# Expert steps of 256 rows with the weights as stationary operand, in a two-layer mixture-of-experts kernel

## The chip, the cores and the metric

The kernel runs on one core of a Trainium2 chip. The metric is the device time of one execution in microseconds (us); lower is better. Times come from executions on the chip. The profile and its trace are of one such execution, and "clock" is the share of full speed that TensorE's throttle granted.
## What is computed

A decayed linear attention, then an expert layer in which each row goes to its best expert, then one in which each row goes to its two best. Cut to what matters:

```python
x = attention(r, k, v, w, u)                     # 3072 rows of 384
e_idx = argmax(x @ w_gate + modality_bias[modality_id])
for e in range(8):                               # layer 0: one expert for each row
    mask = e_idx == e
    h = maximum(x[mask] @ w1[e], 0)              # w1[e] 384 x 1024
    x1[mask] = gate_w[mask, None] * (h @ w2[e])  # w2[e] 1024 x 384
top2 = two best of (x1 @ w_gate2 + softplus(x1 @ w_noise) * noise)
for e in range(8):                               # layer 1: two experts for each row
    for k in range(2):
        mask = top2[:, k] == e
        out[mask] += top2_w[mask, k, None] * (maximum(x1[mask] @ w1b[e], 0) @ w2b[e])
```

Evaluated for the inputs that are timed, the routing sends 2663 and 409 rows to two experts in layer 0 (none to the other six), and 788, 753, 773, 790, 741, 753, 785 and 761 rows to the eight experts of layer 1. Of the first 1536 rows of layer 0, 1336 go to the first expert.

## The kernel before

**Stages.** The attention runs in 24 chunks of 128 tokens. During its last chunks the kernel finds the expert of the first row and lists that expert's rows among the first 1536, so that five tiles of layer 0 (the early tiles, ET = 5) can be gathered before the routing of all rows is known. Then follow layer 0, the gate of layer 1, its routing tables, and layer 1.

**A tile of an expert layer** is 128 rows of one expert, places without a row being filled up. GpSimd gathers the rows with an indirect DMA (`gather_rows`, L551) into one of two buffers `sx`. TensorE transposes them (`slot_turn`, L1556, three 128x128 blocks). VectorE splits the transposed rows into a rounded part `x_hi` and a remainder `x_lo` (`split_x`, L1344, L1346), with two small operations ahead of it in layer 1 for the row's weight (L1339, L1342). A product is three matmuls: hi by hi, hi by lo, lo by hi (`products`, L1644 to L1646), so the weights too are kept as two parts; `split_piece` makes them in four quarters, on ScalarE (L748), VectorE (L1080) and GpSimd (L618), while the first tile of the run before is computed. A run is all tiles of one expert.

**First product** (`up`, L1648): the rows are the stationary operand and 512 columns of w1 stream past, so a half of the hidden values lies in one bank with rows on partitions. There are 2 halves, 3 blocks of 128 inputs and 3 matmuls, 18 matmuls of 512 columns. ScalarE copies the half out (`hidden_copy`, L802), TensorE transposes it in four blocks (`hidden_turn`, L1665), ScalarE applies the ReLU and rounds (`hidden_high`, L807), and VectorE makes the remainder (`hidden_low`, L1351).

**Second product** (`down`, L1668): the hidden values are stationary, and 384 columns of w2 stream past; 8 blocks and 3 matmuls, 24 matmuls of 384 columns. VectorE copies the result out (`result_copy`, L1359 or L1362) and GpSimd scatters it (L654, L657; in layer 1 each scatter adds to the output and waits for the one before).

**Order on TensorE.** `slot_step` (L1697) does for tile s: the first half of `up` for tile s + 1, the first half of `down` for s, `hidden_turn`, the second half of `up`, `slot_turn` for tile s + 2, the second half of `down`, `hidden_turn`. Ahead of it the sequencer reads two entries of the table `slot_run` (`lookup`, L358), whose values set the weights' addresses in both products; the address registers of `weights[:, bass.ds(at, width)]` are computed between the matmuls (PEldq rows of L1644 and L1645). Every engine runs the same steps in `pairs` (L317): some of them written out, then a loop over four steps (L324), then a loop (L1721) in which each step stands under a condition (L1723) since the number of tiles is known only at run time.

**VectorE in the first tiles.** Between the splits of the first tiles VectorE does the routing of layer 0 in small chained operations: `first_counts`, `first_places`, `first_tiles`, `first_slots`, `first_hot` (three parts), `run_order`, `run_experts`, `first_rows`, `slot_tables`, spread over tiles 0 to 2 (`first_step`, L1389).

Of the kernel before, what the change touches and what calls it, by code (L numbers as in the profile page):

```python
# [16 lines left out]
F32 = mybir.dt.float32  # L17
# [7 lines left out]
P = 128  # L25

def attention_moe_moe(nc, HP, D, w_T, kv_T, small_T, modality_T, modality_bias, w1_1, w2_1, w1_2, w2_2, out):
# [15 lines left out]
    ET, EC, EB = 5, 12, 2  # L44
    NS = [N // P + E - 1 + ET, 2 * N // P + E - 1]
    SURE = [K * N // P for K in TOPK]
    NSX = [n + 4 for n in NS]
    NIN = 3
# [5 lines left out]
    assert ET <= EC <= (B - EB) * NC and ET + 3 <= SURE[0] and EB * NC == 12  # L54
# [4 lines left out]
    with ctx:  # L59
# [8 lines left out]

        y_dram = nc.dram_tensor("moe_rows", [N + NSX[0] * P, CX], F32, kind="Internal").ap()

# [9 lines left out]
        iota_s_row_b, iota_row_b = sb("iota_s_row_b", [P, NSX[1]], BF16), sb("iota_row_b", [P, P], BF16)  # L80
        spare_row = [sb(f"spare_row{l}", [P, NSX[l]]) for l in range(2)]
# [14 lines left out]
        with ExitStack() as early:  # L96
            y_tok = [early.enter_context(nc.sbuf_tensor(f"y_tok{i}", [P, C], F32)) for i in range(2)]
            block_ones = early.enter_context(nc.sbuf_tensor("block_ones", [P, P], F32))

        gx_hi = [sb(f"gx_hi{i}", [P, CC, P], F32R) for i in range(NGT)]  # L100
        gx_lo = [sb(f"gx_lo{i}", [P, CC, P], F32R) for i in range(NGT)]
        gate_split = sb("gate_split", [P, CC, 4 * E], F32R)
# [16 lines left out]
        which = sb("which", [P, NSX[1], 2])  # L119
        row_mix = sb("row_mix", [P, NSX[1]])  # L120
        row_mix2 = sb("row_mix2", [P, 2])
# [11 lines left out]
        with nc.sbuf_tensor("logits_T", [4 * E, GB * P], F32) as logits_T:  # L133
            pass
        low_hot = sb("low_hot", [P, 2 * G, P], BF16)
        high_is = sb("high_is", [P, 2 * G, NSX[1]], BF16)
        high_hot = sb("high_hot", [P, 2 * G, 2, NSX[1]], BF16)
        slot_cmp = sb("slot_cmp", [P, NSX[1], E])
# [27 lines left out]
        code = sb("code", [P, NSX[1]])  # L166
        empty = sb("empty", [P, NSX[1]])
        second = sb("second", [P, NSX[1]])
        idx_tmp = sb("idx_tmp", [P, NSX[1]])
        src_row = [sb(f"src_row{l}", [P, NSX[l]], I32) for l in range(2)]  # L170
        dst_row = [sb(f"dst_row{l}", [P, NSX[l]], I32) for l in range(2)]
# [11 lines left out]
        src_now = [sb(f"src_now{i}", [P, 1], I32) for i in range(2)]  # L183
        dst_now = [sb(f"dst_now{i}", [P, 1], I32) for i in range(2)]
# [36 lines left out]
        sx = [sb(f"sx{i}", [P, CX]) for i in range(2)]  # L221
# [1562 lines left out]
```

## Time and profile before

| | |
|---|---|
| median of 3 executions | 1068.34 us (1067.96 to 1069.35) |
| the profiled execution: time, span of its trace | 1067.66 us, 1065.9 us |
| mean granted clock | 0.952 |
| TensorE busy, its loads busy | 960.4 us (90%), 853.7 us (80%) |
| VectorE, ScalarE, GpSimd busy | 529.6 us, 309.3 us, 354.1 us |
| share of the chain that ended last | PE 84%, DVE 8%, issue 3% |
| stages (us from the start) | attention to 178, layer 0 to 443, gate and routing to 528, layer 1 to 1053, end 1065.9 |

The page gives for each group of instructions its line, engine, operation, tiles, count, then busy time, mean duration of one in ns, and the engine's idle time before them with what ended it. Matmuls are pipelined: the duration of one overlaps the next, so what a matmul costs in a row of them is read from the chain that ended last, which gives each only the time by which it moved the chain on. "Issue" is idle time in which an engine waited for nothing that the profile shows; on TensorE it can be its sequencer.

### The profile page before, as it was taken

What the parts mean: (1) busy time and instruction counts of PE and PEld (TensorE: products, weight loads), DVE (VectorE), ACT (ScalarE), POOL (GpSimd) and SP (SyncE); (2) the same over time, 40 slices, a digit from 0 to 9 for tenths busy, and PEclk for the clock granted to TensorE, in tenths of its full rate; (3) what the DMA queues carried; (4) which work ended last, traced back from release to release, by engine and by line L of the source; (5) the groups of instructions that cost most, each with busy time, mean ns of one, the idle gap of its engine ahead of it and who ended that gap; (6) DMA issues with size and microseconds to landing.
All of it is one profiled execution on the core that took longest, in us unless ns stands there. A gap on an engine that the chain in (4) does not pass through costs nothing.

```text
span 1065.9 us, 25001 instructions
## 1 busy us (share of the span) xinstructions
PE 960.4 (90%) x6314; PEld 853.7 (80%) x6315; DVE 529.6 (50%) x915; ACT 309.3 (29%) x537; POOL 354.1 (33%) x420
## 2 busy tenths in 40 slices
PE   6999998999999999382399999999999999999994
PEld 5888887888888898381278988888888988989884
DVE  8889997755323332147753353533535344363231
ACT  2233242223222222042242242423324242332220
POOL 6333334124222222101633343424424333343322
PEclk9999998899999999776599999999999999999998
DMA  6676861082111111153045252342522525222222
GB/s 234 217 217 221 289 233 45 24 306 78 42 45 37 37 44 41 35 171 119 23 150 155 33 160 44 91 101 44 150 42 36 163 38 162 37 37 44 41 35 37
DMA packets 52997, 108.15 MB, mean 101 GB/s; under 512 B 8336, under 2 KB 34704, under 8 KB 52944
## 3 DMA queue, kind: packets, MB, share of 16 engines
q1 hardware_dynamic: 34656, 71.07, 19.6%
q0 software_dynamic: 14400, 31.55, 14.7%
q10 hardware_dynamic: 3888, 4.89, 1.3%
q8 instruction: 25, 0.41, 0.2%
q14 instruction: 28, 0.23, 0.1%
HBM read 82.67 MB, written 24.82 MB: 101 GB/s over the span
## 4 chain that ended last, share of the span: by engine, by line
PE 84%; DVE 8%; issue 3%; DMA 1%; POOL 1%; ACT 1%; ACTq 0%; POOLq 0%; DVEq 0%; SPq 0%
PE ps L1644 21%; PE ps L1646 20%; PE ps L1645 20%; PE ps L1665 6%; PE ps L1556 3%; PE ps L1518 2%; PE ps L1522 2%; PE ps L1487 2%; PE ps L1464 2%; PE ps L1548 2%; DVE row_mix L1339 1%; PE ps L1570 1%; PE ps L1512 1%; PE ps L1581 1%; DVE grow L882 1%
## 5 line engine op out<-in xcount | busy, mean ns | idle before, releaser
L1351 DVE SCALAR_TENSOR_TENSOR hid_lo<-ps,hid_hi 128x512 fp32r<-128x512 f32 x154 | 106.4, 691 | 292.6 <-ACT hid_hi L807 292.5
L1644 PE MATMUL ps<-weights,hid_hi 128*128 (+1 forms) x616 | 215.6, 350 | 8.2 <-issue 6.7
L1644 PE MATMUL ps<-weights,x_hi 128*128 (+1 forms) x462 | 198.2, 429 | 16.1 <-DVE x_lo L1346 8.6
L1646 PE MATMUL ps<-weights,hid_lo 128*128 (+1 forms) x616 | 208.4, 338 | 0.0
L1645 PE MATMUL ps<-weights,hid_hi 128*128 (+1 forms) x616 | 208.3, 338 | 0.0
L1646 PE MATMUL ps<-weights,x_lo 128*128 (+1 forms) x462 | 184.4, 399 | 0.0
L1645 PE MATMUL ps<-weights,x_hi 128*128 (+1 forms) x462 | 184.2, 399 | 0.0
L802 ACT ACTIVATE h_tok<-ps 128x512 f32<-128x512 f32 x154 | 92.3, 599 | 294.8 <-PE ps L1646 284.1
L807 ACT ACTIVATE hid_hi<-ps 128x512 fp32r<-128x512 f32 x154 | 92.1, 598 | 257.7 <-PE ps L1665 257.7
L657 POOL DMA_INDIRECT out_dram<-sy,dst_now x52 | 92.5, 1778 | 210.6 <-DVE sy L1362 199.8
L1644 PEld LDWEIGHTS ps<-weights,hid_hi 128*128 128x128 f32 x616 | 116.7, 190 | 13.5 <-issue 10.3
L1645 PEld LDWEIGHTS ps<-weights,hid_hi 128*128 128x128 f32 x616 | 116.8, 190 | 3.2
L1644 PEld LDWEIGHTS ps<-weights,x_hi 128*128 128x128 f32 x462 | 87.8, 190 | 37.1 <-issue 22.6
L1646 PEld LDWEIGHTS ps<-weights,hid_lo 128*128 128x128 f32 x616 | 116.4, 189 | 0.0
L1646 PEld LDWEIGHTS ps<-weights,x_lo 128*128 128x128 f32 x462 | 88.0, 191 | 20.6
L1645 PEld LDWEIGHTS ps<-weights,x_hi 128*128 128x128 f32 x462 | 88.1, 191 | 14.2
L1665 PE MATMUL ps<-ident,h_tok 128*128 128x128 f32 x616 | 92.8, 273 | 3.4 <-ACT h_tok L802 3.4
L1665 PEld LDWEIGHTS ps<-ident,h_tok 128*128 128x128 f32 x616 | 76.6, 141 | 10.6 <-ACT h_tok L802 3.9
L654 POOL DMA_INDIRECT moe_rows<-sy,dst_now x25 | 26.4, 1057 | 146.4 <-DVE sy L1359 146.4
L551 POOL DMA_INDIRECT sx<-moe_rows,src_now x55 | 56.5, 1027 | 44.0 <-POOL src_now L548 42.3
L748 ACT ACTIVATE weights<-stage 128x1536 f32 (+1 forms) x40 | 59.0, 1481 | 0.0
L1344 DVE CAST x_hi<-ps 128x384 fp32r<-128x384 f32 x79 | 43.7, 553 | 25.0 <-PE ps L1556 25.0
(281 smaller groups left out, 1151.9 us busy)
## 6 DMA issues: line engine op xcount, KB each, us to landing
stage<-in_moe_w_dram SPq DMA_DIRECT2D x18, 1536.0 KB, 9.4
kv_in<-in_kv_T_dram SPq DMA_DIRECT2D x24, 512.0 KB, 5.7
kv_in<-in_kv_T_dram SPq DMA_DIRECT2D x24, 448.0 KB, 3.5
w_in<-in_w_T_dram SPq DMA_DIRECT2D x24, 258.5 KB, 4.4
out_dram<-zeros SPq DMA_DIRECT2D x25, 192.0 KB, 6.6
x_rows<-y_tok ACTq DMA_DIRECT2D x24, 192.0 KB, 5.2
stage<-moe_rows SPq DMA_DIRECT2D x6, 768.0 KB, 4.6
stage<-in_moe_w_dram SPq DMA_DIRECT2D x2, 768.0 KB, 7.0
```

What stands on the lines that cost most here:

```text
L551: pool.indirect_dma_start(out=sx[u][:, 0:width], out_offset=None, in_=rows, in_offset=bass.IndirectOffsetOnAxis(ap=src_now[u][:, :].bitcas ...
L657: pool.indirect_dma_start(out=out, out_offset=where, in_=sy[u][:, 0:C], in_offset=None, compute_op=ALU.add).then_inc(s_scatter[l][u], 16)
L748: act.activation(weights[:, bass.ds((n % 2) * 4 * WSZ + hi + at, HALF)], raw[:, at:at + HALF], ACT.Copy)\
L802: act.activation(h_tok[:, half * FC // 2:(half + 1) * FC // 2, :], h_ps[half], ACT.Copy)\
L807: act.activation(hid_hi[:, half * FC // 2:(half + 1) * FC // 2, :], hT_ps[half], ACT.Relu)\
L1344: dve.tensor_copy(x_hi[:, :, :], sxT_ps).then_inc(s_xhi[l], 1)
L1351: dve.scalar_tensor_tensor(hid_lo[:, part, :], hT_ps[half], 0.0, hid_hi[:, part, :], ALU.max, ALU.subtract).then_inc(s_hlo[l], 1)
L1556: last = pe.transpose(sxT_ps[:, c, :], sx[u][:, c * P:(c + 1) * P], ident[:, :])
L1644: pe.matmul(out_ps, hi, w_hi, start=first, stop=False)
L1645: pe.matmul(out_ps, hi, w_lo, start=False, stop=False)
L1646: return pe.matmul(out_ps, lo, w_hi, start=False, stop=final)
L1665: last = pe.transpose(hT_ps[half][:, m, :], h_tok[:, half * FC // 2 + m, :], ident[:, :])
```

## The change

A step is now 256 rows (TS = 2 tiles of 128), and the early tiles are three steps (ES = 3, six tiles of 128).

- **First product.** The blocks of w1 are the stationary operand (128 inputs by 128 hidden columns) and the transposed rows of both tiles stream past, 256 columns. The result has hidden columns on partitions, as the second product needs it: `hidden_copy`, `hidden_turn` and the tile `h_tok` go. `up` comes in four quarters `q`, each 2 blocks, 3 inputs' blocks and 3 matmuls; a step has 72 matmuls of 256 columns. Its addresses are constants, so the whole body stands twice in the program, for runs with an even and an odd number, each under a condition on `run_next % 2`.
- **Second product.** As before for each tile of 128, into two banks; the second tile's share stands under a condition on a new table `full`, which is 0 when that tile has no row. `up` is done for 256 rows in any case.
- **Order on TensorE.** Per step: `up` quarter 0 of step s + 1, first half of `down` for the second and then the first tile of s, quarters 1 and 2, `slot_turn` of the first tile of s + 2, quarter 3, second half of `down` for the second tile, `slot_turn` of the second tile of s + 2, second half of `down` for the first tile. The body reads three table entries: `slot_run[s]`, `full[s]`, `slot_run[s + 1]`.
- **Buffers.** `x_hi` and `x_lo` hold 256 rows in one copy: `split_x` waits until all four quarters of the step before are done (`s_h`). The transposed rows use one bank, so the second tile's `slot_turn` waits for the first tile's `split_x` (`s_sxc`). ScalarE's `hidden_high` waits for the half of `down` that reads the same part of `hid_hi` (`s_o`).
- **GpSimd.** Two gathers and two scatters per step; in layer 1 the second scatter waits for the first to land.
- **Routing.** Places, slots and tables are counted in steps of 256; the code tables have two columns for each step. VectorE's order in the first steps changes: `first_hot`, `run_order` and `run_experts` all come ahead of `split_x` of step 2.

The core of the diff:

```diff
+                def up(s, q, run, odd=0):
+                    base = odd * 4 * WSZ + W1_HI
+                    pe.wait_ge(s_lov[l], 2 if isinstance(s, int) and s == 0 else run * 3 + 3)
+                    pe.wait_ge(s_sxc[l], s * TS + TS)
+                    if not isinstance(s, int) or s > 0:
+                        pe.wait_ge(s_hlo[l], (s - 1) * 4 + q + 1)
+                    for a in range(2):
+                        for c in range(CC):
+                            at = base + c * F + (2 * q + a) * P
+                            last = products(h_ps[q][:, a, :], weights[:, at:at + P], weights[:, at + WSZ:at + WSZ + P],
+                                            x_hi[:, c, :], x_lo[:, c, :], c == 0, c == CC - 1)
                     last.then_inc(s_h[l], 1)
-                def hidden_turn(s, half, before=None):
+                def down_second(s, half, run, two):
+                    down_ready(s, half, run)
+                    if two is None:
+                        down(s, half, run, 1)
+                    else:
+                        with pe.If(two > 0):
+                            down(s, half, run, 1)
...
+                    run, two, run_next = run_of(s), second_of(s), run_of(s + 1)
+                    def whole(odd):
...
+                            up(s + 1, 0, run_next, odd)
+                            down_second(s, 0, run, two)
+                            down(s, 0, run, 0)
+                        up(s + 1, 1, run_next, odd)
+                        up(s + 1, 2, run_next, odd)
+                        slot_turn(l, s + 2, j + 1, u, 0)
+                        up(s + 1, 3, run_next, odd)
+                        down_second(s, 1, run, two)
+                        slot_turn(l, s + 2, j + 1, u, 1)
+                        down(s, 1, run, 0)
+                    if early(s + 1):
+                        whole(0)
+                    else:
+                        with pe.If(run_next % 2 < 1):
+                            whole(0)
+                        with pe.If(run_next % 2 > 0):
+                            whole(1)
...
+                def split_x(s, u, t):
+                    part = slice(t * P, (t + 1) * P)
+                    dve.wait_ge(s_sxT[l], s * TS + t + 1)
+                    if not isinstance(s, int) or s > 0:
+                        dve.wait_ge(s_h[l], s * 4)
...
                 def first_step(s, u):
+                    if s == 0:
                         first_hot(0)
+                        first_hot(1)
+                        hidden_low(1, 0)
+                        first_hot(2)
+                        hidden_low(1, 1)
                         run_order()
                         run_experts()
...
+                    split_x(s + 2, u, 0)
+                    split_x(s + 2, u, 1)
+                    result_copy(s, s // 2, u)
```

## Rows read from the trace of the kernel before

**Rows 1.** Windows of the two layers: us, busy and count by engine, clock, DMA.

```profile
189.00:443.00 254.00, 243.26 (x1326) 217.84 (x1325) 99.20 (x195) 64.71 (x103) 65.11 (x100) 0.97 0.21 71
546.00:1053.00 507.00, 494.97 (x2700) 442.71 (x2698) 211.96 (x378) 157.69 (x230) 184.53 (x211) 1.00 0.34 77
```

**Rows 2.** The page's groups of instructions: products, transposes, scatters of both layers.

```profile
L1644 PE MATMUL ps<-weights,hid_hi 128*128 (+1 forms) x616 | 215.6, 350 | 8.2 <-issue 6.7
L1644 PE MATMUL ps<-weights,x_hi 128*128 (+1 forms) x462 | 198.2, 429 | 16.1 <-DVE x_lo L1346 8.6
L657 POOL DMA_INDIRECT out_dram<-sy,dst_now x52 | 92.5, 1778 | 210.6 <-DVE sy L1362 199.8
L1665 PE MATMUL ps<-ident,h_tok 128*128 128x128 f32 x616 | 92.8, 273 | 3.4 <-ACT h_tok L802 3.4
L654 POOL DMA_INDIRECT moe_rows<-sy,dst_now x25 | 26.4, 1057 | 146.4 <-DVE sy L1359 146.4
```

**Rows 3.** The chain that ended last, inside layer 1: start, us, what.

```profile
594.99 0.23 PE ps L1645
...
596.16 0.33 PE ps L1556 x3
...
596.67 0.18 PE ps L1645
...
598.61 0.44 PE ps L1665 x4
```

**Rows 4.** Timeline of the stationary loads behind a transpose: start, duration, instruction.

```profile
703.69 0.19 PEld L1644 LDWEIGHTS ps<-weights,x_hi 128*128 128x128 f32 x1
703.80 0.19 PEld L1645 LDWEIGHTS ps<-weights,x_hi 128*128 128x128 f32 x1
```

**Rows 5.** Timelines of VectorE around one split of the rows in layer 1.

```profile
596.65 0.16 DVE L1339 TENSOR_TENSOR row_mix<-sx,which 128x2 f32<-128x2 f32 x1 [1.24 <-PE ps L1556]
...
597.62 0.56 DVE L1346 TENSOR_TENSOR x_lo<-ps,x_hi 128x384 fp32r<-128x384 f32 x1
```

**Rows 6.** Timelines of ScalarE and TensorE, and between them the sequencer's lookups (L358).

```profile
596.20 0.60 ACT L802 ACTIVATE h_tok<-ps 128x512 f32<-128x512 f32 x1 [1.51 <-PE ps L1646]
...
L358 PEldq TENSOR_LOAD <-slot_run x2: 299/300/300, 597.0 to 597.7; - x2
...
598.87 0.49 PE L1644 MATMUL ps<-weights,x_hi 128*128 x1
```

**Rows 7.** By line, the sequencer's address computations (590.1 to 591.1) and branches (428 to 436).

```profile
L1645 PEldq FUSED_REGOPS  x4: 46/46/46, 590.2 to 591.0; - x4
...
L1723 PEldq COMPARE_BRANCH  x12: 208/208/210, 428.9 to 434.9; - x12
```

**Rows 8.** What TensorE waited for in layer 0 (first row) and layer 1.

```profile
PE ps L1644 <- issue: 9.0, 7, 6.7
...
PE ps L1644 <- DVE x_lo L1346: 7.0, 6, 1.2
PE ps L1644 <- issue: 3.5, 11, 0.8
PE ps L1644 <- DVE hid_lo L1351: 1.5, 1, 1.5
```

**Rows 9.** Windows around two waits of TensorE; the clock is the third number from the end.

```profile
236.00:240.00 4.00, 2.39 (x14) 1.85 (x13) 0.00 (x0) 2.38 (x4) 1.21 (x3) 1.00 1.07 394
...
188.50:195.00 6.50, 6.00 (x17) 4.76 (x18) 5.64 (x21) 0.63 (x2) 1.36 (x3) 0.50 0.12 30
```

**Rows 10.** A window of layer 0's first tiles: busy time by engine.

```profile
190.50:216.50 26.00, 25.75 (x147) 23.03 (x148) 19.57 (x53) 6.84 (x11) 4.58 (x7) 0.91 0.10 32
```

**Rows 11.** The instruction fetches of one engine on the page: packets, MB, share.

```profile
q8 instruction: 25, 0.41, 0.2%
```

**Rows 12.** GpSimd in the routing of layer 1; issues of its scatters, median us to landing.

```profile
510.27 5.60 POOL L611 TENSOR_TENSOR high_hot<-high_is,tile_no 128x1416 bf16<-128x1416 bf16 x1 [1.57 <-DVE high_is L1299]
...
out_dram<-sy,dst_now POOLq DMA_INDIRECT x52, 4.4
```

More of the change, by code:

```diff
@@ L165, in attention_moe_moe @@
         split_later = [sb(f"split_later{l}", [P, NSX[l]], I32) for l in range(2)]
[L166 to L171, printed above, removed]
+        full = [sb(f"full{l}", [P, NSX[l]], I32) for l in range(2)]
+        code = sb("code", [P, NTX[1]])
+        empty = sb("empty", [P, NTX[1]])
+        src_row = [sb(f"src_row{l}", [P, NTX[l]], I32) for l in range(2)]
+        dst_row = [sb(f"dst_row{l}", [P, NTX[l]], I32) for l in range(2)]
         index_b, first_idx = sb("index_b", [P, 1], BF16), sb("first_idx", [P, 1])
@@ L1382, in _ @@
                     loop_ends(1)
-                    hidden_low(0, 0)
-                    split_x(1, 1)
-                    hidden_low(0, 1)
+                    for q in range(3):
+                        hidden_low(0, q)
+                    split_x(1, 1, 0)
+                    hidden_low(0, 3)
+                    split_x(1, 1, 1)
                     dve.wait_ge(s_table[1], 3)
@@ L1648, in up @@
-                def up(s, half, run, before=None):
-                    base = (run % 2) * 4 * WSZ + W1_HI + half * (F // 2)
-                    pe.wait_ge(s_lov[l], 2 if before is None else run * 3 + 3)
-                    pe.wait_ge(s_sxc[l], s + 1)
-                    if before is not None:
-                        pe.wait_ge(s_hc[l], before * 2 + half + 1)
-                    for c in range(CC):
-                        last = products(ps[:, 3 + half, :], x_hi[:, c, :], x_lo[:, c, :],
-                                        base + c * F, F // 2, c == 0, c == CC - 1)
-                    last.then_inc(s_h[l], 1)
@@ L1660, in hidden_turn @@
-                def hidden_turn(s, half, before=None):
-                    pe.wait_ge(s_hc[l], s * 2 + half + 1)
-                    if before is not None:
-                        pe.wait_ge(s_hlo[l], before * 2 + half + 1)
-                    for m in range(FC // 2):
-                        last = pe.transpose(hT_ps[half][:, m, :], h_tok[:, half * FC // 2 + m, :], ident[:, :])
-                    last.then_inc(s_hT[l], 1)
-                def down(s, half, run):
-                    base = (run % 2) * 4 * WSZ + W2_HI
+                    return 0 if early(s) else lookup(pe, slot_run[l], s, E - 1)
@@ new lines, in down @@
+                def down(s, half, run, t):
+                    base = (run % 2) * 4 * WSZ + W2_HI
+                    for m in range(half * FC // 2, (half + 1) * FC // 2):
+                        part = slice(t * P, (t + 1) * P)
+                        last = products(o_ps[t], hid_hi[:, m, part], hid_lo[:, m, part],
+                                        weights[:, bass.ds(base + m * C, C)], weights[:, bass.ds(base + WSZ + m * C, C)],
+                                        m == 0, m == FC - 1)
+                    if t == 0:
+                        last.then_inc(s_o[l], 1)
```

425 lines of the change are left out of this document (218 added, 207 removed).

## The prediction

> **What bounds the kernel now.** I read the windows first: in both layers TensorE is busy for 96% and 98% of the stretch, and no other engine for half [rows 1]. The groups then say how much work that is [rows 2]: 616 and 462 matmuls of each kind are 77 tiles (24 x 3 and 18 x 3 for each, 616 transposes make 8), and the scatters split them in 25 and 52. Mean durations are of no use, since matmuls overlap; the chain gives what each costs in a row of them [rows 3]: 0.233 us for 512 columns, 0.175 for 384, 0.33 for the three transposes of new rows, 0.44 for four of hidden values. A tile is 18 x 0.233 + 24 x 0.175 + 2 x 0.44 + 0.33 = 9.6 us, and 77 of them are 740 of the 761 us of the two windows. So the layers are bound by what TensorE is given, and little is lost between tiles: in layer 1 it waits 12 us [rows 8].
>
> **Part 1, TensorE's work.** All is set against the profiled execution, 1067.7 us (span 1065.9 and 1.8 around it), which is 0.7 under the median. The transposes of hidden values go: 77 x 0.88 = **-67.8 us**. The first product keeps its columns for 256 rows (72 x 256 as 36 x 512). No row shows 256 columns. From 512 to 384 the cost falls in proportion (0.455 and 0.456 ns a column), so 256 give 0.1165 us if loading stays hidden. The bound on the other side is the load: two loads behind a transpose start 0.11 us apart [rows 4], so it fits with 0.006 us to spare. I take 0.1165; if load and stream share anything, 0.125 to 0.13 (over 41 x 72 = 2952 matmuls +25 to +40 us), and nothing makes it cheaper than its columns. A step is then 8.4 us of first product. How many steps: the row counts give 11 and 2 in layer 0, and 4, 3, 4, 4, 3, 3, 4, 3 in layer 1, so 13 and 28. That is 82 tiles' worth of first product for 77: 5 x 4.2 = **+21 us**, since 788, 773, 790, 785 and 2663 rows leave a last step with its second tile empty. The second product stays at 77 tiles. Row transposes: 79 turns become 86, **+2.3**.
>
> **Part 2, the wait between steps.** TensorE's sequencer takes its instructions in order, and a semaphore that isn't there stops it. The rows show it: ScalarE's copy ends at 596.80, the lookups, which stand behind the `hidden_turn` that waits for this copy, begin at 597.0, and the next `up` starts at 598.87 [rows 6]: 2.07 us, two lookups of 0.75 in it. Now that time is just covered by the work queued ahead. In the new order the last wait of a step is `slot_turn` of the second tile. It needs the first tile's `split_x`, which now starts only when quarter 3 is done. Between the end of the transposes (596.16 + 0.33) and the end of `x_lo` (597.62 + 0.56) lie 1.69 us [rows 3, 5]; that is the delay from quarter 3 to this wait in layer 1, and without the two small operations about 1.3 in layer 0. From there the sequencer still has to do: the 2.07 of before; a third lookup, 0.75; the addresses of 12 matmuls, 8 computations at half of the 0.27 us between two of L1645, 1.1 [rows 7]; one branch taken and one not, 0.6 (twelve taken ones and six loop ends fill 428.9 to 434.9 and a bit, 0.38 each; the other I take at 0.22). Sum 4.5 us. What TensorE has meanwhile: second half of `down` twice, 4.2, and 0.33, less the 0.17 by which a next matmul starts before the chain's end (598.87 against 598.61 + 0.44). So it stands still for 1.7 + 4.5 - 4.35 = **1.9 us** at each full step of layer 1, and 1.5 in layer 0. Behind the stopped sequencer everything of TensorE is queued, and ScalarE and VectorE wait for it in turn. Below, this could be nothing, if address computations and lookups went on past an open wait; above, 2.5 if the branches over the long bodies cost more.
>
> Layer 1 has 22 such places (28 steps less the last and the 4 partial ones, and one at the start that has its own order), layer 0 has 8, since its first steps have constant addresses and no lookup: 22 x 1.9 + 8 x 1.5 = **+54 us**. A step without second tile is worse: `slot_turn` comes straight behind quarter 3 and TensorE waits the whole 1.9 us for the split, and then has only 0.33 + 2.1 against 4.5 us, another 2.1. Four times 4.0 and once 3.4: **+19.5**. Loop ends and the conditions of the last loop: **+3.5**.
>
> The Trainium skill, Perfetto Trace Analysis (Tensor Engine Instruction), says that the sequencer can fetch the next instruction once one is pushed into the wait queue, ahead of its semaphores. By that rule the lookups would run under the open wait, this part would be near 0, and the kernel would come to the time of the first rival. The trace speaks against it: the lookups begin only behind the copy's end.
>
> **Part 3, waits that go.** Today's waits at run changes and loop ends go or are in the new figures [rows 8]: 7.0 + 3.5 + 1.5 in layer 1, and in layer 0 9.0 less the 6.7 of its end, and 1.6 for `h_tok` [rows 2]: **-16**. The quarters of the new weights are split in steps twice as long and are off the path; if GpSimd's share slows VectorE they cost 1 us each time, eight times, which I leave to the range.
>
> **Part 4, starts and ends.** Layer 0: VectorE does 19.6 us of work in 26 us [rows 10], most of it routing, and nearly all of it now stands ahead of `split_x` of step 2, which `slot_turn` waits for with half of step 0's `down` behind it. TensorE has about 11 us in that stretch: a stall of 6 us, with the clock at half after it; against that the waits of now and 6.5 us at half clock [rows 9] are there today too. I take +5. A second gather and split ahead of the first `up`: +1 and +1.5. Routing of layer 1: code tables of 70 columns for 59, GpSimd's product 5.6 x 70/59, twice in a row in part [rows 12]: +2.6. The second scatter at the end waits for the first to land, 4.4 [rows 12]; between the layers +1.1. The last step's lookups behind empty loop turns: +3.7 and +0.8. Layer 1's first steps wait less for VectorE: -3. Sum **+17**.
>
> **Sum.** -67.8 + 21 + 2.3 + 54 + 19.5 + 3.5 - 16 + 17 = +33.5, or 1101 us; I say **1102**.
>
> **The rivals.** *Hidden boundaries* (the other side: faster). If the sequencer computes past an open wait, or the chain of 4.5 us is in truth under 2.8, the 54, some 8 of the 19.5 and the 3.5 go: 1102 - 65 = 1037, and with half of it 1070. It decides at 4.5 - 1.9 = 2.6 us: a boundary below that costs nothing. For it speaks that today's 2.07 us are fully covered; against it that five things stand in the chain, each from a row. The change is a gain if the stall is under 0.8 us a step.
>
> *The load binds.* Each stationary block now serves 256 columns instead of 512. With 0.125 to 0.13 us a matmul 1127 to 1142. For it: only 0.006 us of slack; against it: at 384 columns no trace of the load is left.
>
> *The clock falls.* A wait of 1.6 us (4.00 less 2.39 busy) left it at 1.00, while behind several waits close together it was 0.50 for 6.5 us [rows 9]. Stalls of 1.9 us, and two of 2 us around 2.4 us of work in the partial steps, lie between the two. If it fell at every third of 38 boundaries for 3.4 to 6.8 us, each 1.5 to 3 us lost, that is +20 to +40: 1122 to 1142. The Trainium skill, TensorE: Matmul & The Clock Gate (The HAM clock gate), has the clock go down only behind an idle stretch; by that it would stay at full speed; rows 9 agree for one wait and leave open what several do.
>
> *Code that must be fetched.* Each step's body now stands twice and each step jumps over one of them. Today 25 fetches bring 0.41 MB, and no jump shows one [rows 11, 7]. If 15 jumps in 38 met code that isn't there, at 1 to 2 us, +15 to +30: 1117 to 1132. The Trainium skill, Advanced Engine Details and Errata (ISA Cache), gives TensorE 128 KB in blocks of 256 instructions; by my count of some 700 instructions a step a loop of four steps would not fit, so it speaks for this case.
>
> **How the numbers follow.** Stalls as computed 0.42 (1085 to 1118); stalls and one of the three costs on top 0.28 (1112 to 1150); boundaries half hidden 0.12 (1066 to 1085 for a quarter of it, 1050 to 1066 for the rest); boundaries hidden 0.16 (1030 to 1050); the rest 0.02. The range that leaves 2 in 10 out is 1045 to 1145. A measurement of this kernel can tell 0.2%, 2 us, from no change. Faster 0.23, within it 0.02, slower 0.75.
>
> **What would show it.** In the profile after: no group for `h_tok`; first-product matmuls 0.117 us apart on the chain (0.125 or more: the load); 82 x 36 of them; TensorE in layer 1 waiting about 1.9 us at each boundary, put down to issue, with the first matmul of `up` quarter 0 behind it; at partial steps a wait for `x_lo` too; clock near 1.00 in both layers; fetches near twice 25, not many times; a longer end by 4 us. I am wrong if the waits put down to issue in layer 1 are under 20 us in sum (then the sequencer runs past waits), if matmuls of 256 columns cost clearly more than their columns, or if VectorE or ScalarE ends the waits in full steps.

## The result and the profile after

The changed kernel takes 1208.6 us (median of 4 runs, 1203.3 to 1211.6) against 1068.2 for the one before, measured beside it: 1.132 times as long, 95% interval 1.127 to 1.137. I had forecast 1102, with a range of 1045 to 1145. The profiled execution took 1211.6 us, with a span of 1209.6.

First the two layers by windows (columns: stretch, its length, busy time and count of TensorE, its weight loads, VectorE, ScalarE and GpSimd, then granted clock, DMA share, GB/s). The stretches go from the first wait of layer 0 to its last product, and from layer 1's first product to its last boundary:

```profile
207.38:463.92 256.54, 218.50 (x1450) 214.05 (x1450) 85.49 (x169) 32.05 (x51) 60.29 (x77) 0.92 0.22 72
552.84:1186.04 633.20, 508.86 (x3384) 496.90 (x3385) 225.82 (x429) 102.51 (x140) 186.92 (x170) 0.91 0.31 70
```

The same stretch of layer 1 took 520.3 us before (from 528.55 to 1048.80). So of the 143.7 us that the span grew by, 113 lie in layer 1, 21 up to the end of layer 0, 3 in the routing between them and 6.5 at the end. TensorE's busy time in layer 1 looks unchanged (505.7 and 508.9), but it is now 80% of the stretch and not 97%, and the clock stands at 0.91 where it was 0.99 ([rows 1] are this reading of before, in a slightly shorter stretch). At half clock a matmul counts twice: half of the busy time at 0.50 is 3.8 us of it before and 36.6 after. Without that TensorE has 29.6 us less to do, close to what Part 1 gives for layer 1 (52 x 0.88 us of transposes gone, four half steps of 4.2 us more: 29.0).

What TensorE waited for (us in total, times, longest; the first rows), beside [rows 8]:

```profile
PE ps L1676 <- issue: 126.6, 33, 10.2
PE ps L1588 <- DVE x_lo L1364: 21.7, 12, 5.5
```

"Issue" was 9.0 and 3.5 us before. The profile shows no engine that TensorE waited for there; that it is TensorE's own sequencer is read from the sequencer's rows further down. On the page of the profile, the fetches of instructions and the first product's matmuls (x984 for each of three, 82 tiles' worth, as counted):

```profile
q8 instruction: 108, 1.77, 0.6%
...
L1676 PE MATMUL ps<-x_hi,weights 128*128 128x256 f32 x984 | 300.2, 305 | 129.8 <-issue 119.2
```

108 fetches for 25 [rows 11]. Between one back edge of the loop in layer 1 and the next there are 11 to 13 of them, in each of the four passes after the first; in the kernel before there are none. The chain of work shows one boundary between steps (start, us, what); it is a mild one:

```profile
936.77 0.18 PE ps L1678
936.95 1.59 issue
938.53 0.38 PE ps L1676
938.91 0.12 PE ps L1677
```

TensorE stands for 1.59 us. VectorE's timeline and the sequencer's rows show what it stood for:

```profile
933.54 0.56 DVE L1364 TENSOR_TENSOR x_lo<-ps,x_hi 128x384 fp32r<-128x384 f32 x1
```

```profile
L1769 PEldq COMPARE_BRANCH  x1: 362/362/362, 935.2 to 935.2; - x1
...
L362 PEldq TENSOR_LOAD <-slot_run x2: 301/306/312, 935.8 to 937.3; - x2
...
L362 PEldq TENSOR_LOAD <-full x1: 302/302/302, 936.5 to 936.5; - x1
```

The split ends at 934.10; from there the sequencer computes addresses, branches at 935.2, makes three lookups until 937.9, branches again and issues at 938.53: 4.43 us, as the prediction's chain of 4.5 has it. But of 35 boundaries that show as a gap, only 16 look like this, idle for 0.7 to 2.0 us. Eighteen are idle for 3.65 to 10.23 us and one for 2.68. (The expectations below measure from the start of the last matmul to the start of the next, 0.34 us more: 3.99 to 10.57, 3.02 and 1.0 to 2.3. The first of them counts 30 boundaries, and puts all nineteen into the first range.) One of the eighteen on TensorE's timeline, with the wait ahead in brackets, and the sequencer's branch in it:

```profile
888.60 0.34 PE L1678 MATMUL ps<-weights,hid_lo 128*128 x1
894.33 0.58 PE L1676 MATMUL ps<-x_hi,weights 128*128 128x256 f32 x1 [5.39 <-issue]
```

```profile
L328 PEldq COMPARE_BRANCH  x1: 3725/3725/3725, 887.4 to 887.4; - x1
```

A branch that takes 0.07 to 0.52 us elsewhere takes 3.73 us here, with a fetch of 16 KB on the instruction queue at 888.4. After 185 us TensorE's sequencer executes 188 branches; 21 of them last over 0.6 us and together 76.0 us. Before there were 50, and none was over 0.25. And the clock ahead of that branch and behind it (third number from the end):

```profile
880.00:887.00 7.00, 7.00 (x55) 6.97 (x55) 2.04 (x6) 0.50 (x1) 0.00 (x0) 1.00 0.01 2
891.23:898.06 6.83, 3.73 (x17) 3.74 (x18) 0.06 (x1) 0.00 (x0) 2.61 (x3) 0.50 0.33 37
```

A stretch at 0.50 begins within 5.3 us of the start of each of the eighteen long gaps, and behind only four of the seventeen shorter ones. Adding up TensorE's busy time in all stretches at 0.50 and taking half of it as lost gives 67.2 us for this kernel and 22.2 for the one before: 45 us.

### The profile page after: what moved, and what is told of

It reads as the page before. It is cut to its first block, busy times and chain, and to the rows that moved or that the text cites. A ratio compares the mean times of both kernels' runs of the same rounds, so it can differ in the third digit from the quotient of the medians.

```text
span 1209.6 us, 23517 instructions
## 1 busy us (share of the span) xinstructions
PE 964.3 (80%) x7285; PEld 922.6 (76%) x7286; DVE 541.7 (45%) x956; ACT 220.0 (18%) x393; POOL 361.1 (30%) x364
## 4 chain that ended last, share of the span: by engine, by line
PE 73%; DVE 12%; issue 11%; DMA 2%; DVEq 1%; POOL 1%; ACT 0%; POOLq 0%; ACTq 0%
PE ps L1676 19%; PE ps L1677 18%; PE ps L1678 18%; PE ps L1588 2%; DVE hid_lo L1369 2%; PE ps L1548 2%; PE ps L1552 2%; PE ps L1517 2%; PE ps L1494 2%; PE ps L1579 1%; PE ps L1602 1%; DVE grow L890 1%; PE ps L1542 1%; PE ps L1613 1%; DVE x_lo L1364 1%
## 5 line engine op out<-in xcount | busy, mean ns | idle before, releaser
L1676 PE MATMUL ps<-x_hi,weights 128*128 128x256 f32 x984 | 300.2, 305 | 129.8 <-issue 119.2
L1676 PEld LDWEIGHTS ps<-x_hi,weights 128*128 128x128 f32 x984 | 201.4, 205 | 142.9 <-issue 136.3
L1678 PE MATMUL ps<-x_hi,weights 128*128 128x256 f32 x984 | 291.6, 296 | 1.7 <-issue 1.7
L1677 PE MATMUL ps<-x_lo,weights 128*128 128x256 f32 x984 | 291.8, 297 | 0.0
L1676 PE MATMUL ps<-weights,hid_hi 128*128 (+1 forms) x616 | 217.0, 352 | 10.4 <-issue 7.4
L1677 PE MATMUL ps<-weights,hid_hi 128*128 (+1 forms) x616 | 212.2, 344 | 1.3 <-issue 1.3
L1677 PEld LDWEIGHTS ps<-x_lo,weights 128*128 128x128 f32 x984 | 202.4, 206 | 0.0
L1678 PEld LDWEIGHTS ps<-x_hi,weights 128*128 128x128 f32 x984 | 201.8, 205 | 0.0
L1676 PEld LDWEIGHTS ps<-weights,hid_hi 128*128 128x128 f32 x616 | 121.1, 197 | 11.2 <-issue 11.2
L1677 PEld LDWEIGHTS ps<-weights,hid_hi 128*128 128x128 f32 x616 | 120.4, 195 | 0.0
L1088 DVE TENSOR_TENSOR weights<-stage,weights 128x1536 f32 (+1 forms) x30 | 61.3, 2068 | 34.3 <-ACT weights L761 31.5
L557 POOL DMA_INDIRECT sx<-moe_rows,src_now x62 | 65.9, 1063 | 35.5 <-POOL src_now L553 24.9
L1588 PE MATMUL ps<-ident,sx 128*128 128x128 f32 x258 | 43.8, 280 | 30.0 <-DVE x_lo L1364 21.7
L1588 PEld LDWEIGHTS ps<-ident,sx 128*128 128x128 f32 x258 | 31.4, 143 | 35.0 <-DVE x_lo L1364 15.3
```

The costliest lines, as they stand in the source:

```text
L557: pool.indirect_dma_start(out=sx[u][:, t, 0:width], out_offset=None, in_=rows, in_offset=bass.IndirectOffsetOnAxis(ap=src_now[u][:, t:t + ...
L1088: dve.tensor_tensor(weights[:, bass.ds(to + lo, HALF)], raw[:, at:at + HALF], weights[:, bass.ds(to + hi, HALF)], ALU.subtract).then_inc(s ...
L1588: last = pe.transpose(x_T[:, c, :], sx[u][:, t, c * P:(c + 1) * P], ident[:, :])
L1676: pe.matmul(out_ps, hi, by_hi, start=first, stop=False)
L1677: pe.matmul(out_ps, hi, by_lo, start=False, stop=False)
L1678: return pe.matmul(out_ps, lo, by_hi, start=False, stop=final)
```

## The experiments

Two theories stood. **Code:** both bodies of four steps don't fit where TensorE keeps its code, so the loop is fetched anew on each pass, and the clock falls behind the waits. **Sequencer:** the stall of 1.6 to 2 us at the other boundaries is the chain that I had added up. Rivals were that a jump over a long body costs wherever the code lies, that weights or splits are late, and that lookups are slow in themselves.

### A shorter loop

```diff
-            twos = (n // 2 - peel) // 2
+            twos = (n // 2 - peel) // per
...
-                for d in range(2):
-                    step(q * 2 + (peel + d), 0)
-                    step(q * 2 + (peel + d), 1)
+                for d in range(per):
+                    step(q * per + (peel + d), 0)
+                    step(q * per + (peel + d), 1)
...
-                pairs(pe, SURE[l] - 2, slot_step, PEEL[l])
+                pairs(pe, SURE[l] - 2, slot_step, PEEL[l], 1)
```

> The changed kernel, with TensorE's loop over the surely used steps holding two steps instead of four; nothing else differs, and the same steps run. By the trace a step issues about 315 matmuls, loads and register instructions, and each step's body stands twice, so a loop of four is about 2500 instructions (five fetches of 16 KB for each 1300) and a loop of two about 1260. In the changed kernel 19 of the 30 step boundaries lasted 3.99 to 10.57 us, each with fetches of 16 KB just ahead of the restart, the others 1.0 to 2.3 us. Theory (code): the loop of four does not stay in the engine's code store and is fetched again on every pass; with two steps it stays. Then some 15 of the 19 long boundaries become 2.0 us: 15 x 3.7 = 56 us, and most of the 41 us that the half clock cost more than before go too: 1100 to 1125 us, under 60 fetches, nearly all boundaries of layer 1 at 1.4 to 2.3 us. Rival (jump): a jump over a body of 20 KB costs this wherever the code lies: 1205 to 1215 us. Rival (load of weights or splits are late at these places): 1205 to 1215 us too.

Measured: 1144.4 us, 1.075 times the kernel before (1.072 to 1.077), 64 us less than the change. The page and the rows of the loop's back edge:

```profile
q8 instruction: 46, 0.75, 0.3%
```

```profile
L328 PEldq COMPARE_BRANCH  x10: 67/213/225, 640.4 to 1006.6; - x10
```

In the change the same edge reads:

```profile
L328 PEldq COMPARE_BRANCH  x5: 67/3600/4837, 699.8 to 1075.3; - x5
```

Past its second pass the short loop has no fetch between its back edges, where the change has 11 to 13. Nothing but the length of TensorE's loop differs, so the code's size is the cause, and the jump over a body and late weights fall as causes of the long boundaries. The windows (same columns as above) and the waits:

```profile
207.74:454.15 246.41, 212.20 (x1450) 207.48 (x1450) 85.54 (x169) 32.06 (x51) 60.49 (x77) 0.94 0.22 74
543.39:1113.96 570.57, 493.47 (x3385) 480.51 (x3385) 237.46 (x429) 102.57 (x140) 193.65 (x170) 0.96 0.33 77
```

```profile
PE ps L1676 <- issue: 63.4, 32, 6.7
PE ps L1588 <- DVE x_lo L1364: 32.4, 14, 5.5
```

Layer 1 is 62.6 us shorter: 47.2 in gaps between matmuls of over 0.5 us, and 15.4 in the rest, where the half clock by the reckoning above costs 17.6 less. Over both layers the gaps put down to issue and to `hid_lo` are 62 us shorter, as the slow branches are (63): in the change's order the fetches show in full. Against that the waits for `x_lo` are 11 us longer than in the change, since GpSimd held VectorE at four places (see "Both, and the row factors behind the split"). The time is above the range that I had expected, because four branches of 12.7 us in sum still miss, by their places when a copy of the loop is entered first, and the half clock still costs 21.6 us more than before.

### The body once

```diff
-                            last = products(h_ps[q][:, a, :], weights[:, at:at + P], weights[:, at + WSZ:at + WSZ + P],
+                            w1_hi, w1_lo = (gx_hi[0][:, 0, :],) * 2 if l == 1 else (weights[:, at:at + P],
+                                                                               weights[:, at + WSZ:at + WSZ + P])
+                            last = products(h_ps[q][:, a, :], w1_hi, w1_lo,
...
-                    if early(s + 1):
+                    if l == 1 or early(s + 1):
                         whole(0)
```

> The changed kernel, but in layer 1 each step's body stands once: the first product takes a fixed 128x128 block as its stationary operand in place of both halves of w1's blocks, so layer 1's products are not the experts' (layer 0 and all routing are untouched, so the steps are the same). The loop keeps four steps. Theory (code): layer 1 has about 1260 instructions in its loop and no jump over a body: its 15 long boundaries fall to 2 us or a bit less (the two branches, some 0.4 us, go too), the clock stays up: 643 us of layer 1 become 545 to 560, the whole 1110 to 1130; layer 0's 4 long boundaries stay. Rival (jump): the same, so this run with the short loop tells: only if the short loop stays at 1205 and this one falls is it the jump. Rival (weights or splits late): no change, 1205 to 1215.

Measured: 1112.5 us (1.042, 1.038 to 1.047). No branch of layer 1 is over 0.6 us, all four slow ones are in layer 0, which still has its two bodies. Layer 1:

```profile
550.64:1085.25 534.61, 482.64 (x3385) 470.60 (x3385) 235.51 (x429) 102.46 (x140) 189.19 (x170) 0.99 0.35 82
```

That is 99 us less than in the change with a loop of four steps kept, and 36 less than with the short loop: without branches and first passes a full boundary is idle for 0.7 to 1.5 us, and the clock falls twice between the layer's first steps and its end. It is a measuring kernel only, since it leaves out w1 in layer 1; its time is no time of a usable kernel.

### Lookups one step ahead

```diff
-                    run, two, run_next = run_of(s), second_of(s), run_of(s + 1)
+                    if early(s):
+                        run, two, run_next = 0, None, run_of(s + 1)
+                    else:
+                        run = pe.snap(carried_run, min_val=0, max_val=E - 1)
...
+                    def look_ahead():
+                        if not early(s + 1):
+                            pe.reg_mov(carried_run, run_next)
+                            pe.reg_load(carried_two, full[l][0:1, bass.ds(s + 1, 1)])
+                            pe.reg_load(carried_next, slot_run[l][0:1, bass.ds(s + 2, 1)])
...
                         down_second(s, 1, run, two)
+                        look_ahead()
                         slot_turn(l, s + 2, j + 1, u, 1)
```

> The kernel with the short loop, and the three lookups of a step (0.75 us each in the trace of before) made one step ahead, in front of the last transposes of new rows and their wait, into registers that carry the values to the next step. Theory (sequencer): the stall at a boundary is 4.5 us of sequencer work behind that wait less 2.66 us of queued work; without 2.25 us of lookups it is covered. Full boundaries of layer 1 go from 2.0 to 0.3 us or less, those of layer 0 from 1.0 to 1.5 to about 0.2, partial steps keep their wait for the split: 50 to 65 us less than the short loop, so 1040 to 1070. Rival (something else releases the first matmul of a step: the branch, the split of the rows, ScalarE's quarter): boundaries stay at 2 us, and the time is that of the short loop within 10 us.

Measured: 1064.2 us, 0.997 of the kernel before (0.994 to 0.999), 80 less than the short loop alone. A full boundary in its chain:

```profile
675.22 0.17 PE ps L1680
675.39 0.17 PE ps L1681
675.56 0.12 PE ps L1679
675.68 0.12 PE ps L1680
```

No gap at all. The work at the boundary is the same, only its place has changed: the stall was sequencer work behind an open wait. Profile against profile it is 75.7 us, 11 of them clock. The other 65 are the upper end of the 50 to 65 expected, which had left the clock out.

### A bank for the second tile

```diff
-                x_T = first_T_ps if isinstance(s, int) and s == 0 and t == 1 else sxT_ps
+                x_T = turned(l, s, t)
...
                         slot_turn(l, s + 2, j + 1, u, 0)
+                        if own_bank(l, s + 2):
+                            slot_turn(l, s + 2, j + 1, u, 1)
                         up(s + 1, 3, run_next, odd)
                         down_second(s, 1, run, two)
-                        slot_turn(l, s + 2, j + 1, u, 1)
+                        if not own_bank(l, s + 2):
+                            slot_turn(l, s + 2, j + 1, u, 1)
```

> The kernel with the short loop (1144.4 us), lookups where the change has them, but the second tile's new rows are transposed into a PSUM bank of their own, right behind the first tile's and ahead of the last quarter of the first product. Then no wait for VectorE's split stands between the last quarter and the next step's first matmul, which itself waits for both splits. Theory (sequencer behind an open wait): the lookups, branches and addresses now run while 4.2 us of second product are queued, so full boundaries fall from 1.6 to 2.1 us to 0.5 or less, as in the run with early lookups; partial steps have no wait of 2 to 3 us at the transposes, but one of 1 to 2.5 us at the first matmul of the next step (both splits 3.4 us behind the last quarter, or the lookups, over 2.1 us of queued work): 1060 to 1085 us. Rival (the lookups are slow for themselves, wherever they stand): boundaries stay over 1.5 us, 1130 to 1145.

Measured: 1068.5 us (1.003, 1.001 to 1.005), 76 less than the short loop. The lookups stand where they stood; with the wait ahead of them gone, they run under queued work. What is left of issue (63.4 us in the short loop):

```profile
PE ps L1682 <- issue: 17.0, 13, 5.8
```

That shuts out the rival of slow lookups. The waits for `x_lo` remain as expected, now at the first product: 22.5 us in 13 of them.

### Both, and the row factors behind the split

```diff
+                    x_T = turned(l, s, t)
+                    dve.tensor_copy(x_hi[:, :, part], x_T).then_inc(s_xhi[l], 1)
+                    dve.wait_ge(s_xhi[l], s * TS + t + 1)
+                    dve.tensor_tensor(x_lo[:, :, part], x_T, x_hi[:, :, part], ALU.subtract).then_inc(s_sxc[l], 1)
+
+                def mix_x(s, u, t):
                     if l == 1:
                         dve.tensor_tensor(row_mix2[:, t, :].unsqueeze(1), sx[u][:, t, C:CX].unsqueeze(1),
...
                     split_x(s + 2, u, 1)
+                    for t in range(TS):
+                        mix_x(s + 2, u, t)
```

> Short loop, early lookups and two banks together, and VectorE's two small products of the row factors moved behind the splits of both tiles. In the run with early lookups (1064.2 us) five full boundaries of layer 1 still lasted 2.1 us; each has a row-factor product of 2.2 us where others take 0.16, while GpSimd splits a block of w2 for 3.5 us; and nine partial steps or starts waited 2.0 to 3.3 us for the split. Theory (shared access of GpSimd and VectorE): only the product with both operands in SBUF is held, the splits that read PSUM are not, so the five boundaries fall under 0.3 us (-9), their clock falls go (-3), partial steps wait about 1.3 us instead of 2.0 to 3.3 (-8): 1040 to 1052. Rival (GpSimd holds up whatever VectorE does next): the split takes the 2 us in the product's place, 1055 to 1062.

What led to it: the timelines of VectorE and GpSimd in the run with early lookups, at one of its five boundaries with 1.7 to 1.8 us idle (2.1 by the measure of the expectation).

```profile
691.15 2.23 DVE L1356 TENSOR_TENSOR row_mix<-sx,which 128x2 f32<-128x2 f32 x1 [0.89 <-PE ps L1588]
```

```profile
689.84 3.51 POOL L625 TENSOR_TENSOR weights<-stage,weights 128x1536 f32 x1
```

A product of two columns, 0.16 us elsewhere, ends when GpSimd's 3.5 us operation ends (693.35 and 693.38). Measured with the new order: 1031.2 us, 0.965 of the kernel before (0.962 to 0.969), better than the 1040 to 1052 expected. The waits for `x_lo` fall from 31 us in the run with early lookups to 9, so the split did not take the product's place, and the half clock costs 8 us less. The run brings the second bank and the new order together; what each gives is not separated here. Layer 1:

```profile
518.80:1004.86 486.06, 474.79 (x3385) 470.03 (x3385) 229.72 (x431) 102.61 (x140) 191.75 (x171) 0.99 0.39 90
```

### Layer 0's start

```diff
                         hidden_low(1, 1)
+                        split_x(2, 0, 0)
+                        split_x(2, 0, 1)
...
                         run_order()
```

> The run before in this call, and in layer 0's first step the split of step 2's rows stands ahead of the routing operations of VectorE (run order and experts) instead of behind them. Theory (my step on layer 0's start: TensorE waits 5.9 us behind 19 us of routing work): the wait at 207.8 us falls to 1 us or less, and what it delays (routing) has slack: 5 to 7 us less than the run before. Rival: the routing then arrives late, and the wait comes back at the first step that needs its tables or the weights loaded by them: within 2 us of the run before.

Measured: 1029.4 us (0.966, 0.963 to 0.968): 2 us less than the run before, inside its spread. The wait at layer 0's start shrinks from 5.5 to 2.1 us idle (5.9 to 2.4 by the expectation's measure), and one of 2.1 us comes at 248.7 us, a boundary that had none. The rival was mostly right.

### The long loop again

The kernel of "both" with the change's own loop of four steps; its diff is the first one, taken back.

> The run with early lookups, two banks and late row factors (1031.2 us), but with the change's own loop of four steps, some 2500 instructions. Theory (code): the fetches of 16 KB come back, over 100 in all, and with them long boundaries. Under it the fetch and the rest of the sequencer's work at a boundary stand one behind the other, so the part of the 3.7 us that the 4.2 us of queued second product can still cover is hidden: each of the 15 to 19 misses costs 1 to 3 us, 1050 to 1085 us. Rival (a fetch costs its 3.7 us and the clock behind it wherever it falls, queued work or not): 1031 + 70 + 30, 1115 to 1135. Rival (the length of the loop is harmless once no wait stands open ahead of the jump): 1028 to 1036.

Measured: 1080.3 us (1.013, 1.010 to 1.016). 108 fetches as in the change, and 21 slow branches of 76.4 us in sum for 5 of 14.6. That is 62 us more of branch time for 49 us of time, of which the half clock by my reckoning is 11: some 23 us of the fetches hide under queued products once no wait stands ahead, where in the change's order next to nothing did. TensorE's gaps say the same: they grow by 37 us. The back edge is even longer than in the change:

```profile
L328 PEldq COMPARE_BRANCH  x5: 74/4853/4950, 637.3 to 963.0; - x5
```

### Two bodies in the kernel before

```diff
                         run_next = run_of(s + 1)
+                        if l == 1:
+                            with pe.If(run_next % 2 < 1):
+                                body(run_next)
+                            with pe.If(run_next % 2 > 0):
+                                body(run_next)
+                        else:
+                            body(run_next)
+
+                    def body(run_next):
                         up(s + 1, 0, run_next, s)
```

> The kernel before the change (128 rows a tile, 1066 us), with the body of each tile of layer 1 standing twice under a condition on the parity of the next run, as the changed kernel has it; both copies are the same. The loop of four tiles is then about 1240 instructions (155 a tile and copy by the trace). Theory (code): it stays in the code store, so no fetch shows in the loop, and only the branches are new, 0.4 to 0.6 us a tile ahead of work that is just covered today: 0 to 25 us, 1066 to 1090. Rival (a jump over a body costs by itself): 50 tiles at 1 to 3 us, 1110 to 1200.

Measured: 1088.1 us (1.020, 1.017 to 1.023). 30 fetches, none of them between back edges past the loop's second pass, and no slow branch. TensorE now stands a bit at nearly each tile boundary:

```profile
747.22 0.44 PE ps L1665 x4
747.66 0.68 issue
748.34 0.49 PE ps L1644
```

So the cover of [rows 6] was as thin as the prediction took it to be: two branches more on the sequencer and 22 us are lost.

### Two bodies and a loop of eight tiles

> The same, but TensorE's loop in layer 1 holds eight tiles instead of four, some 2480 instructions, as many as the changed kernel's loop; the executed instructions are those of the run before but for fewer loop ends. Theory (code): fetches come back in every pass (60 and more on top of 25), a third to a half of the 46 jumps miss, at 3 to 4 us each, and the clock falls behind some: 60 to 120 us over the run with four tiles. Rival (what made the changed kernel slow is its own order, not the code's size): the same time as the run with four tiles, within 5 us.

Measured: 1117.5 us (1.047, 1.044 to 1.050), 29 us more than with four tiles, with 87 fetches for 30 and 11 to 13 between its back edges. The back edges of TensorE's loop, first with eight tiles and then with four:

```profile
L324 PEldq COMPARE_BRANCH  x5: 67/3712/5040, 620.8 to 982.5; - x5
```

```profile
L324 PEldq COMPARE_BRANCH  x11: 76/211/224, 580.8 to 992.7; - x11
```

So it is the size of the code in the old kernel too, and its own order has no part in it. But I had expected 60 to 120 us: only 7 branches are slow (21.9 us), four back edges and three others. Here a jump passes some 155 instructions, in the change some 315, where 13 jumps inside the steps of layer 1 were slow. No run varied the length of the jump alone, so the reason stays open.

### The row factors in the kernel before

The two small products of `split_x` moved behind its last line, nothing else.

> The kernel before the change, with VectorE's two small products of the row factors moved behind the split of the new rows and nothing else. In its profile six of these products take up to 1957 ns where the others take 160, and TensorE stands 1.33 to 1.51 us at a tile boundary each time. Theory (only the product with both operands in SBUF is held while GpSimd splits a block of w2; the splits read PSUM and are not): the six waits shrink to almost nothing, 6 to 9 us less, 1057 to 1060. Rival (GpSimd holds up whatever VectorE does next): within 2 us of 1066.

Measured: 1062.5 us (0.996, 0.994 to 0.998), 4.4 less and not 6 to 9. VectorE's timeline at the place, before and with the new order:

```profile
615.95 1.87 DVE L1339 TENSOR_TENSOR row_mix<-sx,which 128x2 f32<-128x2 f32 x1 [1.23 <-PE ps L1556]
```

```profile
615.99 0.56 DVE L1338 CAST x_hi<-ps 128x384 fp32r<-128x384 f32 x1 [1.11 <-PE ps L1556]
616.58 0.56 DVE L1340 TENSOR_TENSOR x_lo<-ps,x_hi 128x384 fp32r<-128x384 f32 x1
617.05 0.94 DVE L1342 TENSOR_TENSOR row_mix<-sx,which 128x2 f32<-128x2 f32 x1
```

```profile
614.46 3.52 POOL L618 TENSOR_TENSOR weights<-stage,weights 128x1536 f32 x1 [0.77 <-ACT weights L748]
```

The splits run at their 0.56 us while GpSimd, whose row in the new order is the last one, works from 614.46 to 617.98, and only the product is held. Its remainder comes back in part: six waits of 1.06 to 1.24 us idle before (1.33 to 1.51 by the expectation's measure) become three of 0.54 to 0.64 us at the second product. The Trainium skill, SBUF — State Buffer (Who interferes with whom), says this: a VectorE operation with two inputs in SBUF contends with a GpSimd operation that reads SBUF, and one with at most one such input, outside the modes that use both ports, does not; the order of issue decides who is held. Both timelines agree: the held product ends within 0.03 us of GpSimd's operation.

## Why the prediction was wrong, step by step

**The direction and the machine were right, the size was not.** I forecast +34 us and the change costs +140.

**Part 1 held.** x984 matmuls of each kind, and where the clock is full and the matmuls stand in a row the mean start to start is 118.2 ns against 116.5 predicted. Over 2952 matmuls that is 5 us, where the rival in which the load binds wanted 125 to 130 ns and 25 to 40 us: that rival is dead. (The working has "24 x 3 and 18 x 3" matmuls of each kind in a tile; it is 8 and 6 of each of three kinds, 24 and 18 in all, and the sums use those.)

**Part 2 had the mechanism right, and its sum in part by luck.** The chain behind the last wait measured 4.43 us against 4.5, and taking it away by either of two means gave 76 to 80 us, where my terms for it sum to 77. But 11 of those us are clock, which the terms leave out, and the pieces differ: in the short loop, at the eighteen full boundaries of layer 1 that show as a gap and have no slow branch, TensorE is idle for 1.5 us in the mean, not 1.9, and at five of layer 0 for 1.1, not 1.5. At the partial steps of layer 1 the wait for the split is 1.7 us against 1.9. The weakest link was whether the sequencer goes on past an open wait, as the Trainium skill, Perfetto Trace Analysis (Tensor Engine Instruction), has it. The runs are against it too: in the kernel with one bank the lookups begin behind the split, and with two banks the same lookups are hidden.

**Part 3 took away a wait that came back.** It counted the 7.0 us of waits for `x_lo` in layer 1 of before as gone. Six of them were VectorE products held by GpSimd, and the short loop has four such again, of 3.3 us, behind which TensorE waits 2.7 to 2.8 us each, 11 in sum. (Its 14 waits for `x_lo`, 32 us, are these four, two of 2.3 behind VectorE's own weight split, the 5.5 at layer 0's start, five of 1.2 to 1.7 at partial steps and two of 1.5 and 1.65 in the first steps of the layers.) The prediction had left up to 8 us of this to the range. Five waits of the change, 11.2 us, are put down to `hid_lo`, three of them at full steps. That was one of my signs of being wrong; it is a small part of it.

**Part 4 held within a few us** where it can be read: layer 0's start stall 5.5 us (6), the stretch between the layers 3 us longer (2.6 + 1.1), the end 6.5 us longer (4.4 and the last lookups). Its other terms were not measured singly.

**The step that failed is the term for code that must be fetched, left out of the sum and priced low as a rival.** I gave it 15 branches of 1 to 2 us, 15 to 30 us; it was 21 slow branches with 3.6 us at the median of a back edge, 76 us in sum. No row of before had a price, since no jump there misses, and I took a small one. The count had been there: by my own estimate some 700 instructions a step, 2800 in the loop (2500 by the trace). The Trainium skill, Advanced Engine Details and Errata (ISA Cache), gives 128 KB and 256 instructions to 16 KB, by which I estimate room for 2048; the runs lie on both sides of it, with 1240 and 1260 kept and 2480 to 2520 fetched again. That should have made this the likeliest case, and not one of three costs that shared a chance of 0.28. *The clock* I priced at 20 to 40 us, also outside the sum; it was 45. And I took the costs for separate cases, each alone on top of the forecast, where one brings the other: a stretch at half clock begins behind each of the eighteen long gaps, and with the short loop the half clock costs 23 us less.

**The sum closes to about 10 us.** 1102, and 45 for the clock, and 74 for the slow branches over their usual time, gives 1221; the profiled execution took 1211.6. With the short loop it is 1102 + 21.6 + 12.4 = 1136, against 1139.8, of which 11 are the four held products. So without the added clock loss, the fetches and the held products (two in the change, with waits of 1.7 and 1.8 us) the kernels come to 1089 and 1095, 7 to 13 under my 1102. The shorter stalls (0.4 us at 30 places, less the 5 us of Part 1) would be 7 of that by estimate; the rest stays open.

**What is left of the idea.** The change of layout itself saves time. With a loop that fits, lookups one step ahead, a second bank and the row factors behind the split it is 1031 us, and 2.9% under the kernel before with its own row factors moved (1062.5). That this is near the 1037 of my rival with hidden boundaries is no support for that rival: the sequencer does not run past the wait, its work was moved.

## What to carry to other kernels

Count the instructions of a loop body, for each copy that a branch makes of it, before the work that the branch saves: past a size between 1260 and 2480 on TensorE each pass paid 3.6 to 5.0 us at its back edge, up to 6.5 at a jump inside, and then again in the clock. What a sequencer has to do at a loop or step boundary should stand ahead of the last wait and not behind it: here the lookups behind an open wait did not start, and moving them was worth 76 to 80 us, clock included. And when one rival would bring on another, price them together.

## What was new about the hardware

- A branch into code that must be fetched shows as the branch's own duration: in the change 12 of 21 took 3.5 to 3.84 us and the others 1.2 to 6.2 (6.5 in the long loop of the best kernel), where the rest took 0.07 to 0.52.
- A loop of TensorE that didn't fit was fetched anew on every pass: 11 to 13 fetches of 16 KB for some 2500 instructions, none past the second pass for some 1250.
- A fetch costs less where matmuls are queued and no wait stands open: some 23 of 62 us were hidden then, and about 1 of 63 in the change's order.
- For the same size of loop, 13 jumps of layer 1 over some 315 instructions were slow, and 3 over some 155. The reason stays open.
- GpSimd's 3.5 us operation held a VectorE product of two columns until its own end, for 1.9 us in the kernel before and up to 3.3 in the short loop, and left the splits that read PSUM alone.
